# Attention work in three visits per group, with the first block's scores put into the last visit of the group ahead

## The chip, the cores and the metric

The kernel runs on one core of one Trainium2 chip. The metric is the device time of one execution in microseconds, as the median of several runs. The core has five engines that run their own instruction streams in order and meet at semaphores: TensorE (PE; its weight loads are shown apart as PEld), VectorE (DVE), ScalarE (ACT), GpSimd (POOL) and SyncE (SP), which issues the DMAs here.

## The reference

Three stages follow each other over 3072 tokens: a recurrence with decay (8 heads of 48 channels), a feed-forward stage with a quadratic knee, and a gated feed-forward stage.

```python
# stage 1, r k v w: (4, 8, 768, 48)
for t in range(S):
    cur = einsum('bhd,bhe->bhde', u * kt, vt)
    y[:, :, t] = einsum('bhd,bhde->bhe', rt, state + cur)
    state = wt[..., None] * state + einsum('bhd,bhe->bhde', kt, vt)
x = y.transpose(0, 2, 1, 3).reshape(3072, 384)
# stage 2, w_in (384, 2048), w_out (2048, 384)
h = x @ w_in
g = where(h >= 1, h, where(h <= -1, 0, (h + 1) ** 2 / 4))
x = g @ w_out
# stage 3, gate and val (384, 1536), w_out (1536, 384)
g = x @ w_gate
out = (g * sigmoid(g) * (x @ w_val)) @ w_out
```

## The kernel before, in words

Tokens are worked in `NG` = 8 groups of `T` = 384, each group in `NW` = 3 blocks ("windows") of 128 tokens. The recurrence is turned into matrix products per block. For each block there are, on TensorE:

- `AT`, the scores (line 1497): products of k and r, both scaled by running products of w, into two banks. It is one fill of 32 matmuls for a group from the third on, or 28 and more in others.
- `Y`, the output (lines 1523 and 1528): r against the decayed state (32 matmuls, left out for the first block of a sequence), then the masked scores against v (64 matmuls).
- `ST`, the state update (line 1515): k, turned to token order, against v (32 matmuls, 8 in the last block of a sequence).

Every second group begins a sequence, so its first block has no state. For groups 2 to 7 (`moved(g)`, with `MOVED` = 2), k and the output x are turned by VectorE in 32 x 32 blocks and a DMA through DRAM (`turn_k`, `turn_x`, `move_k`, `move_x`), not by TensorE.

The first feed-forward stage is `phase1`: 8 groups of `J1` = 16 slots. In slot j TensorE does `tile_in` for hidden tile j+2 (nine 128x128 by 384 matmuls, line 1438), then the attention work of the next group that is placed in that slot (a "visit"), then `tile_out` for hidden tile j (nine matmuls, line 1466). Each product of fp32 values is three matmuls of a high and a low part. `win_slots(g)` says which attention fills stand in which slot, and TensorE (`do_fill`), ScalarE and VectorE (`drain`) go through them in the same order.

ScalarE computes the knee's first part of tile j+2 (lines 977, 979) and the high part of tile j+1 (970). VectorE makes in slot j the low part of tile j+1 (`lo`, line 1273) and finishes the knee of tile j+2 (`knee`, line 1280). `tile_out(j)` waits for `lo(j)`, and `tile_in(j)` for `knee(j-2)`. After these two VectorE does the slot's other work, placed by tables: the low part of x (`X_SPLIT_SLOTS`, 1268), the turning of k (`K_BLOCK_SLOTS`, `K_BLOCK_AHEAD`, 1251), the scaling of k and r (`SCALE_SLOTS`, `SCALE_AHEAD`, 1153 and 1156), the sums for the term with u (`DIAG_SLOTS`, 1161), the drains of a visit (Y at 1234, x turned at 1260, state at 1223, decay at 1182, masked scores at 1204), and the scans of w for the group after next (`SCAN_SLOTS`, 1131, 1134, 1141). ScalarE checks w in `CHECK_SLOTS`.

GpSimd makes r*k*u for each block (`diag_products`, lines 848 and 851) and, when VectorE has summed it, its product with v (`diag_values`, 858), which the drain of Y adds. SyncE issues loads and moves in one written order (`attention_of`, `half`), and waits at each for what must come before.

A bank written by `ST` has free columns in which the next block's `AT` may stand, so that `AT` needn't wait for the state drain of the same visit; the drain of `ST` then waits for that `AT` fill. Until now this held for the second and third block of a group only.

Phase 2 (8 groups of 12 slots) holds only feed-forward matmuls.

Of the kernel before, what the change touches and what calls it, by code (L numbers as in the profile page):

```python
# [36 lines left out]
NW = 3  # L37
# [25 lines left out]


MOVED = 2
VISITS_MOVED = [[("AT", 0, 0), ("AT", 0, 1)],
                [("Y", 0, 0), ("ST", 0, 0), ("AT", 1, 0), ("AT", 1, 1)],
                [("Y", 1, 0), ("ST", 1, 0), ("AT", 2, 0), ("AT", 2, 1)],
                [("Y", 2, 0), ("ST", 2, 0)]]
FILLS_MOVED = [f for visit in VISITS_MOVED for f in visit]  # L70
NF, NF_MOVED = len(FILLS), len(FILLS_MOVED)
K_BLOCK_SLOTS = {0: 1, 4: 2}
K_BLOCK_AHEAD = {12: 0}
X_SPLIT_SLOTS = {7: 0, 10: 1, 12: 2}
BLK = 32
NB = P // BLK
MOVE = 16 * NB
# [12 lines left out]
OPS_DIAG = 2  # L90


SCALE_SLOTS = {0: 2}
SCALE_AHEAD = {12: 0, 15: 1}
DIAG_SLOTS = {2: 0, 4: 1, 5: 2}
def visits_at(slots, visits, order):
    return {j: tuple(order.index(f) for f in visit) for j, visit in zip(slots, visits)}


WIN_SLOTS = visits_at((1, 3, 6, 8), VISITS_MOVED, FILLS_MOVED)  # L100
WIN_FIRST = visits_at((4, 6, 7, 9, 10, 12, 13), VISITS, FILLS)
XT_FIRST = 13

CHECK_SLOTS = {4: 0, 7: 1, 10: 2}
CHECK_AHEAD_FIRST = {9: 0, 10: 1, 12: 2}
SUM_SLOT = 14
SCAN_SLOTS = {5: 0, 9: 1, 11: 2}


CHECK_FIRST = {0: 1, 3: 2}  # L110
# [12 lines left out]
def first(g):  # L123
    return isinstance(g, int) and g == 0


def win_slots(g):
    return WIN_FIRST if first(g) else WIN_SLOTS


def check_slots(g):
# [19 lines left out]
def fill_no(g, kind, w, n=0):  # L151
    return fills(g).index((kind, w, n))


def build_program(nc, w_d, kr_d, tok_d, u_d, cst_d, w1i_d, w1o_d, w2g_d, w2v_d,
                  w2o_d, rs_d, ks_d, vs_d, ws_d, us_d, out_d, x2_d, ys_d, kb_d, xb_d):
    ctx = ExitStack()
    with ctx:
# [471 lines left out]
        def _(e):  # L630
# [96 lines left out]
            def attention_of(g, loads):  # L727

                def then_load(load, w):
                    if loads:  # L730
                        load(g + 1, w)

                then_load(load_w, 0)
                move_k(g, 1)
                then_load(load_w, 1)
                then_load(load_kr, 0)
                then_load(load_tok, 0)
                move_x(g, 0)
                move_k(g, 2)
                then_load(load_w, 2)  # L740
                move_x(g, 1)
                move_x(g, 2)
                for w in (1, 2):
                    then_load(load_kr, w)
                    then_load(load_tok, w)

            def half(g, after_next):

                if after_next and g == 0:
                    for w in range(NW):  # L750
                        load_kr(2, w)
                        load_tok(2, w)
                elif after_next:
                    attention_of(g + 1, True)
                if after_next:
                    move_k(g + 2, 0)
                wait(M["ea", 1], g * 2 + 4)
                wait(M["ed", 1], g + 2)

                e.dma_start(half_of(x2_d, g), stage[:, :, :]).then_inc(M["st", 1], 16)  # L760
# [56 lines left out]
        @block.gpsimd  # L817
        def _(e):

            e.memset(last[:, :], W_TOT_LEAST).then_inc(zero_p, 1)  # L820
            e.wait_ge(zero_p, 1)
            e.memset(last[:, WIN::SEG], 1.0).then_inc(zero_p, 1)
            e.memset(seed[:, :], 0.0).then_inc(zero_p, 1)
            e.memset(st[:, :, :], 0.0).then_inc(zero_p, 1)
            for i in range(2):
                for n in range(2):
                    e.memset(att[i][n][:, :, :], 0.0).then_inc(zero_p, 1)
            e.memset(sbar[1][:, :, :], 0.0).then_inc(zero_p, 1)
            e.memset(sbar[0][:, :, :], 0.0).then_inc(st_dec, OPS_DECAY)

            def split_lo(c, src, raws, lo, whi_s, wlo_s):
                n = len(raws)
                e.wait_ge(whi_s, c + 1)
                e.wait_ge(raws[c % n], 16 * (c // n + 1))
                e.tensor_tensor(lo[0], src, lo[1].bitcast(F32), ALU.subtract).then_inc(wlo_s, 1)

            def w1_lo(c):
                if c == DVE_CHUNK:
                    return
                t = w1i if c % 2 == 0 else w1o  # L840
                split_lo(c, chunk_raw(c), raw, (t[1][:, c // 2, :], t[0][:, c // 2, :]), whi, wlo)

            def diag_products(g, w):

                n = (g * NW + w) * OPS_DIAG
                rk = r_tok(w)
                e.wait_ge(ld["tok", w], (g + 1) * 16)
                e.tensor_tensor(rk, rk, k_tok(w), ALU.mult).then_inc(diag_p, 1)
                e.wait_ge(diag_p, n + 1)
                e.wait_ge(ld["u"], 16)  # L850
                e.tensor_tensor(rk, rk, uu[:, :], ALU.mult).then_inc(diag_p, 1)

            def diag_values(g, w):

                e.wait_ge(ld["tok", w], (g + 1) * 16)
                e.wait_ge(diag_d, g * NW + w + 1)
                d_b = dg[:, w, :].rearrange("p (h o) -> p h o", o=1).to_broadcast([P, H, D])
                e.tensor_tensor(r_tok(w).rearrange("p (h d) -> p h d", d=D),  # L858
                                v_tok(w).rearrange("p (h d) -> p h d", d=D), d_b, ALU.mult).then_inc(diag_v, 1)

            def decay_second():

                w = 2
                e.wait_ge(scan, OPS_SCAN * w + 1)
                e.wait_ge(st_out, 2 * w)
                e.wait_ge(diag_p, NW * OPS_DIAG)
                for i in range(2):
                    r0, c0 = 64 * i, D * i
                    rows = slice(r0, r0 + D)
                    e.wait_ge(st_dec, OPS_DECAY * w + i * (OPS_DECAY // 2))  # L870
                    wt = suf[rows, w, 0::SEG].rearrange("q (p o) -> q p o", o=1).to_broadcast([D, NPAIR, D])
                    e.tensor_tensor(sbar[twin(0, w)][rows, :, c0:c0 + D], st[rows, :, :], wt, ALU.mult).then_inc(st_dec, OPS_DECAY // 2)
                e.wait_ge(st_dec, OPS_DECAY * (w + 1))

            diag_products(0, 0)
            diag_products(0, 1)
            diag_values(0, 0)
            diag_products(0, 2)
            decay_second()
            diag_values(0, 1)  # L880
            diag_values(0, 2)
            for c in range(2 * J1):
                w1_lo(c)
                if c in PRODUCTS_AT:
                    diag_products(1, PRODUCTS_AT[c])
                if c in VALUES_AT:
                    diag_values(1, VALUES_AT[c])
            for g in range(2, NG):
                for w in range(NW):
                    diag_products(g, w)  # L890
                    diag_values(g, w)
            for c, (j, s) in enumerate(order2):
                lo = w2o[1][:, j, :] if s == 2 else w2gv(1, j, s)
                hi = w2o[0][:, j, :] if s == 2 else w2gv(0, j, s)
                split_lo(c, ring2[:, c % RING2, :], raw2, (lo, hi), whi2, wlo2)
# [226 lines left out]
        def _(e):  # L1122
# [61 lines left out]
            def drain(g, f, parity):  # L1184
# [21 lines left out]
                elif kind == "ST":  # L1206
# [5 lines left out]
                    if moved(g):  # L1212
                        for b in range((n_pair + 1) // 2):
                            if w < NW - 1:
                                e.wait_ge(fill, fills_before(g) + fill_no(g, "AT", w + 1, b) + 1)
                            pairs = slice(2 * b, min(2 * b + 2, n_pair))
                            n_half = pairs.stop - pairs.start
                            for i in range(2):
# [126 lines left out]
            def slot(g, j, parity, next_half, after_next):  # L1345
# [30 lines left out]
                if next_half and not (first(g) and j == XT_FIRST):  # L1376
                    for f in win_slots(g).get(j, ()):
                        drain(g + 1, f, 1 - parity)
                if j == J1 - 1 and first(g):
                    copy_out(1, g)  # L1380
                if after_next:
                    if j in scan_slots(g):
                        scan_window(g + 2, scan_slots(g)[j])
                    if j in SCALE_AHEAD:
                        scale_window(g + 2, SCALE_AHEAD[j])
                    if j in K_BLOCK_AHEAD:
                        turn_k(g + 2, K_BLOCK_AHEAD[j])
                if after_next and j == SUM_SLOT:
                    sum_w(g + 2)
                if j == J1 - 1 and not first(g):  # L1390
# [31 lines left out]
        def _(e):  # L1422
# [114 lines left out]
            def bank_free(g, f):  # L1537

                if moved(g):
                    kind, w, n = fills(g)[f]  # L1540
                    if kind != "Y":
                        e.wait_ge(st_out, states_done(g * NW + w - (1 if kind == "AT" and w > 0 else 0)))
                    if kind == "ST":
                        e.wait_ge(at_out, (g * NW + w + 1) * 2)
                        return
# [50 lines left out]
            def slot(g, j, parity, next_half, after_next):  # L1596
# [10 lines left out]
                if next_half:  # L1607
                    for f in win_slots(g).get(j, ()):
                        do_fill(g + 1, f, 1 - parity)
                tile_out(1, g, j, w1o)  # L1610

            phase1(e, slot)
# [82 lines left out]
```

## Time and profile before

| | us |
|---|---|
| median of 3 runs | 955.07 |
| lowest, highest | 953.28, 956.41 |
| the profiled execution | 953.63 |
| its span, first to last instruction | 951.8 |
| PE busy in it | 933.3 (98%) |
| DVE busy | 548.2 (58%) |
| ACT busy | 392.2 (41%) |
| POOL busy | 173.4 (18%) |

The profiled execution has 1.8 us around its span. Phase 1 with the attention work takes the first half of it (to about 450 us), phase 2 the rest.

How to read the views: "busy" adds up the time in which an engine had an instruction running; "idle before" is the time just before it, with what ended it (the releaser). "issue" is time in which the engine waited for nothing that the profile shows. In the chain of waits each piece is a run of instructions of one line on the path that ended last.

### The profile page before, as it was taken

The page shows a single profiled execution, that of the slowest core. Times are in us where ns is not written, and L with a number is a line of the kernel's source. Part 1 is how long each engine was busy: PE and PEld are TensorE (multiplying, and loading weights), DVE is VectorE, ACT ScalarE, POOL GpSimd, SP SyncE. Part 2 cuts the span into 40 slices and gives each one's busy share as a digit, 9 for nine tenths or more (in the row PEclk, how much of TensorE's full clock was granted, in tenths as well). Part 3 has the DMA queues.
Part 4 walks back from the last instruction along what each step waited for, and adds up shares of the span by engine and source line. Part 5 has one row for each costly group of instructions (what it writes and reads, how often), then busy time and mean ns, then how long its engine had stood idle before and what let it go on. Part 6 is the DMA issues. An engine that isn't in the chain of part 4 may idle for free.

```text
span 951.8 us, 20721 instructions
## 1 busy us (share of the span) xinstructions
PE 933.3 (98%) x8344; PEld 917.5 (96%) x8344; DVE 548.2 (58%) x975; ACT 392.2 (41%) x827; POOL 173.4 (18%) x155
## 2 busy tenths in 40 slices
PE   6899999999999999999999999999999999999998
PEld 5889999999999999999999999999999999999997
DVE  8998877877777778774444433334343343434333
ACT  5675545455554545535664222222222222222222
POOL 6993220402204022021444100000000000000000
PEclk9999999999999999999999999999999999999999
DMA  9824443344433444212324010010101001010000
GB/s 311 247 83 179 139 135 127 113 148 131 142 123 118 142 134 132 110 58 92 108 84 131 3 51 1 1 51 1 51 0 50 0 0 50 0 50 0 25 1 27
DMA packets 49715, 79.58 MB, mean 84 GB/s; under 512 B 14784, under 2 KB 35648, under 8 KB 49632
## 3 DMA queue, kind: packets, MB, share of 16 engines
q1 hardware_dynamic: 49632, 78.42, 25.2%
q8 instruction: 58, 0.95, 0.4%
q14 instruction: 25, 0.20, 0.1%
HBM read 60.71 MB, written 17.69 MB: 82 GB/s over the span
## 4 chain that ended last, share of the span: by engine, by line
PE 93%; DVE 4%; issue 1%; ACT 0%; DMA 0%; DVEq 0%
PE bank L1438 51%; PE bank L1466 36%; PE bank L1497 2%; PE bank L1528 2%; PE bank L1523 1%; DVE suf L1131 1%; PE bank L1515 1%; DVE k_r_by_channel L1156 0%; DVE k_r_by_channel L1153 0%; DVE att L1198 0%; DVE gate L1280 0%; DVE glo L1273 0%; DMA w_by_channel<-in_w_channel 0%; DVE diag L1161 0%; DVE w_by_channel L1141 0%
## 5 line engine op out<-in xcount | busy, mean ns | idle before, releaser
L970 ACT ACTIVATE ghi<-gate 128x384 fp32r<-128x384 f32 x224 | 117.3, 524 | 207.4 <-DVE gate L1292 95.4
L1273 DVE TENSOR_TENSOR glo<-gate,ghi 128x384 fp32r<-128x384 f32 x224 | 136.6, 610 | 83.6 <-ACT ghi L970 81.8
L1290 DVE TENSOR_TENSOR gate<-bank,gate 128x384 f32<-128x384 f32 x96 | 53.5, 558 | 215.0 <-ACT gate L1091 215.0
L1438 PE MATMUL bank<-xhi,w2gv_ahi 128*128 128x384 f32 x480 | 161.3, 336 | 0.0
L1438 PE MATMUL bank<-xlo,w2gv_ahi 128*128 128x384 f32 x480 | 161.3, 336 | 0.0
L1438 PE MATMUL bank<-xhi,w2gv_alo 128*128 128x384 f32 x480 | 161.3, 336 | 0.0
L1091 ACT ACTIVATE gate<-bank 128x384 f32<-128x384 f32 x96 | 47.2, 492 | 227.7 <-PE bank L1438 227.7
L1466 PE MATMUL bank<-ghi,w1ohi 128*128 128x384 f32 x384 | 132.7, 346 | 0.9 <-DVE glo L1273 0.9
L1438 PE MATMUL bank<-xhi,w1ihi 128*128 128x384 f32 x384 | 129.5, 337 | 1.4 <-issue 0.9
L1438 PE MATMUL bank<-xhi,w1ilo 128*128 128x384 f32 x384 | 129.4, 337 | 0.0
L1466 PE MATMUL bank<-glo,w1ohi 128*128 128x384 f32 x384 | 129.4, 337 | 0.0
L1438 PE MATMUL bank<-xlo,w1ihi 128*128 128x384 f32 x384 | 129.2, 337 | 0.0
L1466 PE MATMUL bank<-ghi,w1olo 128*128 128x384 f32 x384 | 129.2, 337 | 0.0
L1280 DVE SCALAR_TENSOR_TENSOR gate<-bank,gate 128x384 f32<-128x384 f32 x128 | 71.0, 555 | 73.4 <-ACT gate L979 72.7
L1466 PE MATMUL bank<-ghi,w2ohi 128*128 128x384 f32 x288 | 96.8, 336 | 0.0
L1466 PE MATMUL bank<-ghi,w2olo 128*128 128x384 f32 x288 | 96.8, 336 | 0.0
L1466 PE MATMUL bank<-glo,w2ohi 128*128 128x384 f32 x288 | 96.8, 336 | 0.0
L977 ACT ACTIVATE gate<-bank 128x384 f32<-128x384 f32 x128 | 62.6, 489 | 82.7 <-PE bank L1438 82.7
L1438 PEld LDWEIGHTS bank<-xhi,w2gv_ahi 128*128 128x128 f32 x480 | 90.2, 188 | 0.0
L1438 PEld LDWEIGHTS bank<-xlo,w2gv_ahi 128*128 128x128 f32 x480 | 90.2, 188 | 0.0
L1438 PEld LDWEIGHTS bank<-xhi,w2gv_alo 128*128 128x128 f32 x480 | 90.2, 188 | 0.0
L858 POOL TENSOR_TENSOR r_k_v_by_token<-r_k_v_by_token,diag 128x384 f32<-128x384 f32 x24 | 27.7, 1155 | 270.9 <-DVE diag L1161 270.8
(105 smaller groups left out, 1550.3 us busy)
## 6 DMA issues: line engine op xcount, KB each, us to landing
r_k_v_by_token<-in_rkv_token SPq DMA_DIRECT2D x21, 672.0 KB, 6.1
k_r_by_channel<-in_kr_channel SPq DMA_DIRECT2D x18, 512.0 KB, 4.9
w_by_channel<-in_w_channel SPq DMA_DIRECT2D x24, 226.2 KB, 3.2
k_blocks_out<-k_blocks SPq DMA_DIRECT2D x18, 256.0 KB, 2.1
k_moved<-k_blocks_out SPq DMA_DIRECT2D x72, 64.0 KB, 2.0
x_t<-ring SPq DMA_DIRECT2D x8, 576.0 KB, 3.2
x_raw<-x_t SPq DMA_DIRECT2D x8, 576.0 KB, 4.0
ring<-in_w_out SPq DMA_DIRECT2D x21, 192.0 KB, 2.8
```

The costliest lines, as they stand in the source:

```text
L858: e.tensor_tensor(r_tok(w).rearrange("p (h d) -> p h d", d=D), v_tok(w).rearrange("p (h d) -> p h d", d=D), d_b, ALU.mult).then_inc(diag_v, 1)
L970: e.activation(ghi[j % 2][:, :], gate[j % 2][:, :], ACT.Copy).then_inc(M["hi", ph], 1)
L977: e.activation(q, hid[j % 2][:, 0:T], ACT.Relu, bias=0.5, scale=0.5).then_inc(M["q", 1], 1)
L1091: e.activation(gate[j % 2][:, :], hid[j % 2][:, 0:T], ACT.Sigmoid).then_inc(M["q", 2], 1)
L1131: e.tensor_tensor_scan(suf[:, w, ::-1], w_at[:, w, :0:-1], last[:, ::-1], 0.0, ALU.mult, ALU.max).then_inc(scan, 1)
L1273: e.tensor_tensor(glo[j % 2][:, :], gate[j % 2][:, :], ghi[j % 2][:, :].bitcast(F32), ALU.subtract)\
L1280: e.scalar_tensor_tensor(q, hid[j % 2][:, 0:T], 1.0, q, ALU.max, ALU.min).then_inc(M["g", 1], 1)
L1290: e.tensor_tensor(q, hid[j % 2][:, 0:T], q, ALU.mult).then_inc(M["t", 2], 1)
L1438: m = e.matmul(out, w_of(a, k), x_of(b_, k), start=start and i == 0, stop=stop and i == total - 1)
L1466: m = e.matmul(acc[k][:, 0:T], wo[a][:, j, k * P:(k + 1) * P], gs[b_][:, :], start=(j == 0 and i == 0), stop=(j == J[ph] - 1 and i == 2))
L1497: m = e.matmul(o[a:a_end, p * WIN + t:(p + 1) * WIN], kr[r, w, 0, p, t:t_end], kr[r, w, 1, p, t:], start=True, stop=True)
L1528: m = e.matmul(out[t, h * D:(h + 1) * D], att[twin(g, w)][h % 2][:, h // 2, t], v_of_scores(g, w, h), start=(row_start and h == 0), stop=( ...
```

## The change

The visits to attention of groups 2 to 7 are placed anew. Before, they stood at slots 1, 3, 6 and 8 of the group ahead: the first scores alone; Y, ST of block 0 with scores 1; Y, ST of block 1 with scores 2; Y, ST of block 2. Now they stand at slots 2, 5 and 8, and the scores of the first block of groups 3 to 7 follow Y and ST of the last block of the group before them, in its visit at slot 8. Group 2 has no such visit ahead, so its first scores stand alone, at slot 0 instead of slot 1.

Around it:
- the drain of `ST` of a group's third block waits for the next group's first `AT`, and that `AT` no longer for the third block's state drain (`joined`);
- the scaling, the turning and the move of the first block's k come earlier: slot 6 and 7 instead of 12, and on SyncE between the moves of x of blocks 1 and 2 instead of at the end;
- the third block's scaling is at slot 1 (was 0), the sums at 1, 3, 6 (were 2, 4, 5), the splits of x at 6, 9, 12 (were 7, 10, 12), the checks at 3, 7, 10 (were 4, 7, 10), the scans at 4, 10, 13 (were 5, 9, 11);
- GpSimd makes all three blocks' products of a group before the first of its values.

```diff
-VISITS_MOVED = [[("AT", 0, 0), ("AT", 0, 1)],
-                [("Y", 0, 0), ("ST", 0, 0), ("AT", 1, 0), ("AT", 1, 1)],
+FIRST_SCORES = [("AT", 0, 0), ("AT", 0, 1)]
+VISITS_MOVED = [[("Y", 0, 0), ("ST", 0, 0), ("AT", 1, 0), ("AT", 1, 1)],
                 [("Y", 1, 0), ("ST", 1, 0), ("AT", 2, 0), ("AT", 2, 1)],
                 [("Y", 2, 0), ("ST", 2, 0)]]
-FILLS_MOVED = [f for visit in VISITS_MOVED for f in visit]
+FILLS_MOVED = FIRST_SCORES + [f for visit in VISITS_MOVED for f in visit]
-K_BLOCK_AHEAD = {12: 0}
-X_SPLIT_SLOTS = {7: 0, 10: 1, 12: 2}
+K_BLOCK_AHEAD = {7: 0}
+K_BLOCK_AHEAD_FIRST = {12: 0}
+X_SPLIT_SLOTS = {6: 0, 9: 1, 12: 2}
-SCALE_SLOTS = {0: 2}
-SCALE_AHEAD = {12: 0, 15: 1}
-DIAG_SLOTS = {2: 0, 4: 1, 5: 2}
+SCALE_SLOTS = {1: 2}
+SCALE_AHEAD = {6: 0, 15: 1}
+SCALE_AHEAD_FIRST = {12: 0, 15: 1}
+DIAG_SLOTS = {1: 0, 3: 1, 6: 2}
-WIN_SLOTS = visits_at((1, 3, 6, 8), VISITS_MOVED, FILLS_MOVED)
+WIN_SLOTS = visits_at((2, 5, 8), VISITS_MOVED, FILLS_MOVED)
+WIN_SECOND = {0: (0, 1), **WIN_SLOTS}
+SCORES_AHEAD = 8
-CHECK_SLOTS = {4: 0, 7: 1, 10: 2}
+CHECK_SLOTS = {3: 0, 7: 1, 10: 2}
-SCAN_SLOTS = {5: 0, 9: 1, 11: 2}
+SCAN_SLOTS = {4: 0, 10: 1, 13: 2}
...
+def scores_ahead(g, j):
+    return g + 1 >= MOVED and g + 2 < NG and j == SCORES_AHEAD
...
@@ SyncE, attention_of(g, loads)
                 move_x(g, 1)
+                if loads:
+                    move_k(g + 1, 0)
                 move_x(g, 2)
...
@@ GpSimd
             for g in range(2, NG):
                 for w in range(NW):
                     diag_products(g, w)
+                for w in range(NW):
                     diag_values(g, w)
...
@@ VectorE, drain of ST
                             if w < NW - 1:
                                 e.wait_ge(fill, fills_before(g) + fill_no(g, "AT", w + 1, b) + 1)
+                            elif g + 1 < NG:
+                                e.wait_ge(fill, fills_before(g + 1) + fill_no(g + 1, "AT", 0, b) + 1)
...
@@ VectorE, slot
+                if scores_ahead(g, j):
+                    for n in range(2):
+                        drain(g + 2, fill_no(g + 2, "AT", 0, n), parity)
...
@@ TensorE, bank_free
-                        e.wait_ge(st_out, states_done(g * NW + w - (1 if kind == "AT" and w > 0 else 0)))
+                        joined = kind == "AT" and g * NW + w > MOVED * NW
+                        e.wait_ge(st_out, states_done(g * NW + w - (1 if joined else 0)))
...
@@ TensorE, slot
+                if scores_ahead(g, j):
+                    for n in range(2):
+                        do_fill(g + 2, fill_no(g + 2, "AT", 0, n), parity)
```

## Rows read from the trace of the kernel before

**Rows 1.** The profile's page: span, busy time of each engine, and 40 slices.
```profile
span 951.8 us, 20721 instructions
PE 933.3 (98%) x8344; PEld 917.5 (96%) x8344; DVE 548.2 (58%) x975; ACT 392.2 (41%) x827; POOL 173.4 (18%) x155
...
PE   6899999999999999999999999999999999999998
```

**Rows 2.** Chain of waits, main groups 5 and 6: start us, us, what.
```profile
357.17 0.80 PE bank L1523 x32
...
359.11 0.84 PE bank L1497 x22
359.95 1.77 PE bank L1466 x9
...
368.34 1.76 PE bank L1466 x9
...
396.62 0.81 PE bank L1497 x24
397.43 1.78 PE bank L1466 x9
```

**Rows 3.** Chain of waits, from main group 2's last visit to group 3's first.
```profile
188.35 1.56 PE bank L1438 x9
189.91 0.80 PE bank L1523 x32
...
193.38 1.59 PE bank L1438 x9
...
218.81 1.59 PE bank L1438 x9
...
223.01 1.56 PE bank L1438 x9
```

**Rows 4.** Chain of waits, main group 1's visit at slot 6.
```profile
122.52 0.70 PE bank L1497 x15
123.22 0.51 issue
123.73 0.55 PE bank L1497 x10
```

**Rows 5.** DMA queues in the window from 119 to 126 us: packets, MB, share of engines.
```profile
q8 instruction: 2, 0.03, 1.9%
```

**Rows 6.** TensorE in order of time, main group 4: visits at 3 and 8 begin.
```profile
286.02 0.87 PE L1523 MATMUL bank<-state_decayed,k_r_by_channel 112*32 112x96 f32 x32
...
307.62 0.87 PE L1523 MATMUL bank<-state_decayed,k_r_by_channel 112*32 112x96 f32 x32
```

**Rows 7.** VectorE in order of time, main group 4, slots 3 to 7.
```profile
287.68 0.55 DVE L1234 TENSOR_TENSOR x_by_token<-bank,r_k_v_by_token 128x384 f32<-128x384 f32 x1
...
292.32 0.54 DVE L1273 TENSOR_TENSOR glo<-gate,ghi 128x384 fp32r<-128x384 f32 x1
...
293.82 0.70 DVE L1251 STREAM_TRANSPOSE k_blocks<-k_r_by_channel 128x512 f32<-128x512 f32 x1
...
295.12 1.22 DVE L1273 TENSOR_TENSOR glo<-gate,ghi 128x384 fp32r<-128x384 f32 x1 [0.17 <-ACT ghi L970]
...
298.34 0.55 DVE L1161 TENSOR_REDUCE diag<-r_k_v_by_token 128x8 f32<-128x384 f32 x1 [1.32 <-POOL r_k_v_by_token L851]
298.81 1.22 DVE L1131 TENSOR_TENSOR_SCAN suf<-w_by_channel,last_of_segment 112x516 f32<-112x516 f32 x1
...
301.67 0.53 DVE L1273 TENSOR_TENSOR glo<-gate,ghi 128x384 fp32r<-128x384 f32 x1
...
306.97 0.54 DVE L1273 TENSOR_TENSOR glo<-gate,ghi 128x384 fp32r<-128x384 f32 x1
```

**Rows 8.** GpSimd in order of time, main group 3: the value of block 0.
```profile
226.85 1.24 POOL L858 TENSOR_TENSOR r_k_v_by_token<-r_k_v_by_token,diag 128x384 f32<-128x384 f32 x1 [40.56 <-DVE diag L1161]
```

**Rows 9.** SyncE's DMA issues in order of time, main group 2: block 2's k.
```profile
182.61 3.02 SPq L684 DMA_DIRECT2D k_moved<-k_blocks_out  x4
```

More of the change, by code:

```diff
@@ L127, in win_slots @@
 def win_slots(g):
-    return WIN_FIRST if first(g) else WIN_SLOTS
+    return WIN_FIRST if first(g) else WIN_SECOND if g + 1 == MOVED else WIN_SLOTS
+def scores_ahead(g, j):
+    return g + 1 >= MOVED and g + 2 < NG and j == SCORES_AHEAD
 def check_slots(g):
@@ L754, in half @@
                     attention_of(g + 1, True)
-                if after_next:
-                    move_k(g + 2, 0)
+                if after_next and g == 0:
+                    move_k(2, 0)
                 wait(M["ea", 1], g * 2 + 4)
@@ L1383, in slot @@
                         scan_window(g + 2, scan_slots(g)[j])
[L1384 to L1387, printed above, removed]
+                    scale_ahead = SCALE_AHEAD_FIRST if first(g) else SCALE_AHEAD
+                    if j in scale_ahead:
+                        scale_window(g + 2, scale_ahead[j])
+                    k_ahead = K_BLOCK_AHEAD_FIRST if first(g) else K_BLOCK_AHEAD
+                    if j in k_ahead:
+                        turn_k(g + 2, k_ahead[j])
                 if after_next and j == SUM_SLOT:
```

## The prediction, made before the changed kernel was timed

> **What bounds the kernel now.** I read the page first, then the chain of waits through phase 1, then single visits in order of time. TensorE is busy for 933.3 of 951.8 us, and its row of slices is full from the third slice on [rows 1]. What is missing, 18.5 us, lies almost all in the first 45 us, which the change doesn't touch. So no other engine is the bound. A change to the placing of attention work can gain only in three ways: less lost time where TensorE goes from one kind of tile to another, fewer stalls inside a visit, or a shorter pitch of the large matmuls. In the chain of waits a tile of nine large matmuls takes 1.56 us, and a visit is the same few pieces each time, 0.80 for r against the state and 0.84 for scores among them [rows 2, 3]. Two things in the chain depart from this pattern: stretches in which a tile takes 1.59 us instead of 1.56 [rows 3], and one visit with 0.51 us of "issue" in the middle of its scores [rows 4].
>
> **One visit less.** The first scores cost, alone, their piece of 0.81 us plus a longer first tile after them, 1.78 against 1.56: 0.81 + 0.22 = 1.03 us [rows 2, 3]. The visits with Y pay that longer first tile in any case: 1.76 without scores at the end, 1.77 with them [rows 2]. Joined scores so add 0.84 + 0.01 = 0.85 us. Each join saves 1.03 - 0.85 = **0.18 us**, and there are five (groups 3 to 7): 0.9 us. Group 2's first scores only go from slot 1 to slot 0: nothing gained. The matmuls themselves are all still there. (The Trainium skill, page "TensorEngine Tiling (Array Packing)", section "Key Properties", says that changing the tiling mode drains TensorE. The trace agrees in sign: a join takes away one such change, and 0.18 us is what that is worth here.)
>
> **The pitch.** After main group 2's last visit all 17 tiles up to group 3's first visit take 1.59 us; before the visit, and after the next one, 1.56 [rows 3]. The same happens after group 4's last visit, and for five tiles after the visits at slot 3 in groups 1 and 2: some 44 tiles at 0.03 us, 1.3 us in all. Nothing waits in these tiles. It looks like a phase in which TensorE comes out of a visit and which it keeps until the next. The two long stretches both follow a last visit that ends with ST, two of the six such visits; of the eighteen visits that end in scores two were followed by a slow stretch, a short one. After the change five of the six last visits end in scores. If they come out like those, the two long stretches go: 2 x 17 x 0.03 = **1.0 us**. At 2 in 18 over five stretches of 20 tiles some 0.3 us of that comes back. I take 0.7 us. Bounds: all five slow costs 5 x 20 x 0.03 = 3.0 us against the 1.0 of now, a loss of 2.0; all short stretches fast as well gains 1.3.
>
> **The stall.** Group 1's scores at slot 6 took 0.70 + 0.51 + 0.55 = 1.76 us for 0.84, with no semaphore between their matmuls [rows 4], while instruction blocks and k's small packets were under way [rows 5]. I read it as TensorE waiting for its instructions. The same visit exists after the change, now at slot 5, so I leave it where it is: 0. It can go (a gain of 0.92) or come at other visits (below).
>
> **VectorE.** It loses no work and gets none: its operations change place. The question is where `lo` or `knee` now comes late. After visit 5 is the narrowest place. Take the start of visit 2 as zero and use main group 4's times around its visit at slot 3, which began at 286.02. The drains run from 287.68 to 292.32, that is from +1.7 to +6.3 [rows 6, 7]. In slot 4 the knee of tile 6 is bound by TensorE: `tile_in(6)` ends at 2.8 + 4 x 1.56 + 0.2 = +9.2, and with ScalarE's checks (now in slot 3) the knee is done by about +11.0. The turning of k (0.70) and a scan (298.81 to 301.67, 2.86) follow: +14.6 [rows 7]. With `lo`, `knee` +15.5. The drains of visit 5, 4.64 long: +20.1, then `lo(7)` +20.6. TensorE wants it after two visits of 2.8, ten tiles and twice 0.2: +21.6. So there is 1.0 us to spare. In the kernel before, the like place is after the visit at slot 6: `lo(8)` ended at 307.5, when `tile_in(10)` was just over, and only the visit at slot 8, which began at 307.62, covered it [rows 6, 7]. There VectorE had also waited 1.32 us for GpSimd's product of block 2 [rows 7]; as the products now come before all values, that wait goes. I cost VectorE at 0, covered by 1.0 us after visit 5; from both sides, it can't gain (no wait of TensorE on VectorE is there to remove after 50 us), and each us beyond the cover costs 6 us, one for each group.
>
> After visit 2 `lo(4)` is done by +6.8 and wanted at 2.8 + 0.2 + 4 x 1.56 = +9.2. After visit 8 the drains may first start at +1.6 past its start, `lo(10)` follows at +6.8 and is wanted at +9.2; the scan in slot 10 comes behind it. Both have 2.4 us of cover. At slot 13 the scan stands without k's scaling and turning, which were at 12, so it is no worse than slot 11's now. The scores ahead need k scaled at slot 6: the scaling ends near +23, the scores start near +26.6.
>
> **GpSimd and the sums.** The sum of block 0 moves to slot 1 behind a scaling, ending near zero; GpSimd's value takes 1.24 [rows 8], and the drain of Y wants it at +1.6. That is 0.3 us of cover, with visit 2's 2.4 us behind it. The products of block 2, now queued ahead of the first value, wait for its load, which is issued after x's third move and has some 20 us. (The Trainium skill, page "SBUF — State Buffer", section "SBUF: two separate sides", says that a VectorE operation with two SBUF inputs and a GpSimd operation lock each other out. The trace agrees: a `lo` beside GpSimd took 1.22 us for 0.54 [rows 7]. By that rule every overlap would be worth up to 0.7 us on VectorE, within the cover.)
>
> **SyncE's queue.** The move of block 0's k of the next group now stands ahead of x's third move. It waits for k turned at slot 7 (near +25) and the moved block takes some 4 us from store to the last load; x's third block is turned near +28. Nothing waits behind it yet. In slot distance x's moves have 3 slots and more as before. The third k move follows x's first: in group 2 its loads were issued at 182.61, and the visit at slot 8 that wants them began at 189.91 [rows 3, 9]. From the first visit with Y to that at slot 8 there were five slots and are now six, so its 7.3 us grow by one slot's 3.1. The turning at slot 7, which needs the k buffer free, has about one slot less, some 4 us after the move has landed. Cost 0, covered by that.
>
> **The sum.** 953.63 (951.8 of span and 1.8 around it) - 0.9 - 0.7 = 952.0 for an execution like the profiled one. The median of the three runs lies 1.44 above that execution, so the same change puts the median at 955.07 - 1.6 = **953.4 us**, 0.17% less.
>
> **Rivals.**
> - *Instructions come late at visit 8.* With the scores it has up to 160 matmuls and as many weight loads in 2.8 us, where before it had 128 or fewer pairs. Visits of that size are the ones where the stall [rows 4] happened, once in nine. (The Trainium skill, page "Runtime: NRT & Kernel Launch", section "Instruction fetch mechanics", says that instructions come in blocks of 256; a visit of 320 may cross two blocks. The two instruction packets in that window agree [rows 5].) If all five visits stall for 0.92 us: +4.6 - 1.6 = +3.0, that is 958.1, **slower**. It decides against the change from the second stall on (0.92 x 2 > 1.6). For it: the next group's k now moves at that time, too. Against: eight of nine such visits had none.
> - *VectorE comes late after visit 5.* If the cover of 1.0 is short by 0.3 to 0.8, 6 x = 1.8 to 4.8 us: 955.2 to 958.2.
> - *The pitch goes the wrong way.* All five stretches slow: 955.07 - 0.9 + 2.0 = 956.2.
> - *More goes than I count.* The stall of group 1 (0.92) and all slow stretches (1.3) go with the 0.9: 955.07 - 3.1 = 952.0, **faster** by over 0.3%.
> - *Nothing changes:* joined scores cost what lone ones did, since the free time is that of the bank switch, and the pitch stays: 955.1.
>
> **How the numbers follow.** 0.3% of 955.07 is 2.9 us, about what a measurement of this kernel can tell from none: below 952.2 is faster, above 957.9 slower. The forecast (a gain of 0.9 to 2.4 us) has 0.52, instructions late 0.09, VectorE late 0.10, pitch worse 0.09, more gained 0.12, nothing 0.08. The three runs differ by 3.1 us, which spreads each case by some 1 us: faster takes half of its rival's case and a fifth of the forecast, 0.19; slower takes most of the first and half of the second rival, 0.12; 0.69 for within. The range reaches down to the fourth rival with that spread and up to the first two: 951.2 to 957.2.
>
> **What would show it.** Right: in groups 3 to 7 no scores alone; the piece of scores after ST at slot 8 at 0.81 to 0.85 us with a next tile of 1.76 to 1.79; tiles of 1.56 from visit 8 to visit 2; no wait of TensorE on VectorE after 50 us. Wrong: "issue" within a visit, a wait of line 1466 on `glo` (1273) in slot 7 or of 1438 on the gate (1280), 1.59 us over the long stretches, or a lone 1.3 us of POOL's wait now on VectorE's sums at slot 2.

## The result, and the profile after

| | before | after |
|---|---|---|
| median of 20 runs | 955.08 us | 957.71 us |
| lowest, highest | 952.66, 957.62 | 954.65, 961.05 |
| ratio after to before (95% interval) | | 1.0026 (1.0017 to 1.0035) |
| the profiled execution, its span | 953.63, 951.8 us | 958.64, 956.9 us |

The changed kernel is slower by 2.6 us, where 1.7 us less was forecast. The time lies 0.5 us above the range, whose end was 957.2.

The page has nearly the same busy times as before [rows 1]:

```profile
span 956.9 us, 20723 instructions
PE 935.7 (98%) x8344; PEld 921.0 (96%) x8344; DVE 556.7 (58%) x975; ACT 393.3 (41%) x827; POOL 171.5 (18%) x155
```

The view that settles it is that of the waits of TensorE alone, from 95 to 460 us. Columns: us in total, times, longest. Of the kernel before, the one line was the stall of [rows 4]:

```profile
PE bank L1497 <- issue: 0.5, 1, 0.5
```

After:

```profile
PE bank L1515 <- issue: 3.0, 3, 1.1
```

The matmuls wait for no other engine there; TensorE stops three times in the middle of scores, for "issue". The chain of waits shows them at slot 5 of main group 2, slot 2 of group 4 and slot 8 of group 5:

```profile
180.44 0.81 PE bank L1515 x22
181.25 1.02 issue
182.27 0.27 PE bank L1515 x2
...
286.34 0.83 PE bank L1515 x23
287.17 1.07 issue
288.24 0.33 PE bank L1515 x3
...
370.98 0.82 PE bank L1515 x21
371.80 0.94 issue
372.75 0.34 PE bank L1515 x5
```

Undisturbed, a visit with state, scores, ST and the next scores takes 3.32 us from the start of the last matmul of `tile_in` to that of the second of `tile_out`. These three took 4.58, 4.71 and 4.59: 3.9 us lost, against 0.9 in the one of before (4.24). That is 3.0 us more. The joins stand where they should. Here is the one of main group 4, slot 8, with what follows it:

```profile
311.93 0.20 PE bank L1533 x7
312.13 0.83 PE bank L1515 x24
312.96 1.80 PE bank L1484 x9
314.76 1.59 PE bank L1456 x9
...
343.38 1.59 PE bank L1456 x9
...
348.91 1.56 PE bank L1456 x9
```

The scores add their 0.83 us and no second change of tiles, but all 19 tiles from there to the next visit go at 1.59 us, as 17 did behind group 2 before [rows 3]. In this execution some 66 tiles did so (19 each after groups 4 and 5, 23 after group 6, 5 in group 3), 2.0 us in all, against 1.3 before. From the visit after them on (348.91) a tile takes 1.56 us again.

The two spans differ by 5.1 us: 3.0 of stalls, -0.9 of joins, +0.7 of pitch, and 2.4 us that the first 50 us took longer (the first visit of group 1's attention came at 50.66 instead of 48.22), where both kernels have the same work. That last part differs from execution to execution: the first large tile began at 28.88 in the profile of before and at 30.45 in this one; over the profiles below it lay between 28.9 and 30.0 us, in no order that I can see (but for the one with 140 increments). Without it there remain 2.8 us, and the medians differ by 2.6.

### The profile page after: what moved, and what is told of

Same layout as the page of the kernel before. It is cut to its first block, busy times and chain, and to the rows that moved or that the text cites. A ratio compares the mean times of both kernels' runs of the same rounds, so it can differ in the third digit from the quotient of the medians.

```text
span 956.9 us, 20723 instructions
## 1 busy us (share of the span) xinstructions
PE 935.7 (98%) x8344; PEld 921.0 (96%) x8344; DVE 556.7 (58%) x975; ACT 393.3 (41%) x827; POOL 171.5 (18%) x155
## 4 chain that ended last, share of the span: by engine, by line
PE 93%; DVE 3%; issue 1%; DMA 1%; ACT 1%; SPq 0%; DVEq 0%; ACTq 0%
PE bank L1456 51%; PE bank L1484 36%; PE bank L1515 2%; PE bank L1546 2%; PE bank L1541 2%; PE bank L1533 1%; DMA w_by_channel<-in_w_channel 1%; DVE suf L1142 1%; DVE gate L1293 0%; DVE glo L1286 0%; PE bank L1501 0%; ACT state_decayed L940 0%; DVE k_r_by_channel L1167 0%; DVE w_by_channel L1152 0%; DVE k_r_by_channel L1164 0%
## 5 line engine op out<-in xcount | busy, mean ns | idle before, releaser
L1286 DVE TENSOR_TENSOR glo<-gate,ghi 128x384 fp32r<-128x384 f32 x224 | 141.2, 630 | 82.1 <-ACT ghi L981 80.6
L1484 PEld LDWEIGHTS bank<-ghi,w1ohi 128*128 128x128 f32 x384 | 72.1, 188 | 3.9 <-issue 2.2
```

What stands on the lines that cost most here:

```text
L1286: e.tensor_tensor(glo[j % 2][:, :], gate[j % 2][:, :], ghi[j % 2][:, :].bitcast(F32), ALU.subtract)\
L1484: m = e.matmul(acc[k][:, 0:T], wo[a][:, j, k * P:(k + 1) * P], gs[b_][:, :], start=(j == 0 and i == 0), stop=(j == J[ph] - 1 and i == 2))
```

## Theory and rivals

**Theory: instruction blocks.** All three stalls, and the one of before, have the same place in TensorE's instruction stream. Counting its instructions in the trace (weight loads, matmuls and the few semaphore instructions), they come behind numbers 4544, 7104, 9408 and, before, 3008. All four leave 192 when divided by 256. Over phase 1 of the profile of after the instruction queue moves one packet of 16 KB for each 256 of TensorE's instructions. (The Trainium skill, page "Runtime: NRT & Kernel Launch", section "Instruction fetch mechanics", gives 16 KiB blocks of 256 instructions; the trace agrees. It also says that crossing a boundary is mostly hidden, as instructions are issued more slowly than fetched. In these visits that isn't so: 327 instructions pass in 2.8 us, and the stalls above are measured.) A visit with Y, ST and scores has 327 instructions, so that two ends of blocks can lie in it. The positions of the first end in the four stalled visits were 45 (before), 64, 62 and 58 instructions from the visit's start; the next end comes 256 later, and there the stall is. In two visits of before, groups 2 and 4, the first end stood at 28 and 26, and nothing stalled. My reading: the block after next is asked for when one ends; if that is at the start of a visit, it was asked for while the large matmuls still ran, and if it is deeper in, the 256 instructions of the next block are used up in 2 us, before the new one is there. The instruction packets bear this out: in the three stalled visits they began 0.5, 0.7 and 0.4 us after that end (0.5 in the one of before), in the two unstalled ones 0.9 and 1.2 us ahead of it. From the first end to the end of the stall it took 3.2 to 3.3 us in the three visits of after and 2.8 in that of before. Two views of the DMA queues (packets, MB, share of engines) show it: the stalled visit of after at 178 us has its first end at 179.05, and the packet comes in the 2 us behind it (window from 179.05 to 181.05):

```profile
q8 instruction: 1, 0.02, 4.6%
```

The unstalled visit of before at 181 us has its first end at 180.85, and the packet comes in the 2 us ahead (window from 178.85 to 180.85; the 2 us behind have none):

```profile
q8 instruction: 1, 0.02, 3.0%
```

The visit that stalls is thus a matter of the program's layout, which added or moved instructions change. The joins move it, and three more visits have 327 instructions (twelve instead of nine).

**Rivals.** The new places in the slots cost the time, by waits or pitch. Or: the stalls belong to DMA traffic at that moment. Or: the pitch of 1.59 us is worse since the visits end otherwise.

The theory allows a test that leaves every piece of work in place: put some instructions ahead of TensorE's first fill, where it waits for its first data anyway, and shift all the ends of blocks. Increments of a semaphore that nothing waits for serve as such.

## Experiment 1: the changed kernel, shifted by 62

```diff
+            for _ in range(62):
+                e.sem_inc(HELD["pe"], 1)
             for f in range(NF):
                 do_fill(0, f, 0)
```

> The changed kernel with 62 semaphore increments put ahead of TensorE's first fill; nothing else. Theory (instruction blocks): TensorE's instructions come in blocks of 256, and TensorE stops inside a visit when one block ends 35 to 70 instructions into it and the next ends 256 later, still in the visit. The 62 instructions move every boundary, and no visit is left with two of them in that position: the three stalls of 1.21 to 1.34 us at 181, 287 and 371 us go (3.8 us less), no 'issue' within a visit after 95 us, and the median falls from 957.7 to about 954, 1.1 us below the kernel before. Rival (the placing): the new slots cost it, through waits or the pitch; then the stalls stay in the same visits or the time stays within 1 us of 957.7.

Measured: median 953.25 us (12 runs) against 955.12 of the kernel before on the same chip, ratio 0.9984 (0.9976 to 0.9993). The three stalls are gone, and the changed kernel is now faster than the one before. Group 3's last visit, with its joined scores, in the chain of waits:

```profile
247.38 0.80 PE bank L1541 x32
248.18 0.68 PE bank L1546 x64
248.86 0.45 PE bank L1533 x31
249.31 0.84 PE bank L1515 x22
250.16 1.77 PE bank L1484 x9
```

The new places of the work thus cost next to nothing; the rival of the placing falls. One trace of VectorE's lateness is left: in main group 3, slot 7, TensorE waited for `lo(7)`, and its large matmuls there came 0.26 us late, in this one of the six profiles of the changed kernel:

```profile
PEld bank L1484 <- DVE glo L1286: 0.4, 1, 0.4
```

Behind the 62 increments the first matmul came at 10.7 us, where the changed kernel has it at 7.7, so they outlast TensorE's wait for its first data by 3.0. The first large tile still began at 29.39 us, between the 28.88 and 30.45 of the two kernels without increments, so what was lost at the start was made up by then.

The waits of the weight loads showed a small rest, at two visits with a block's end 77 and 79 instructions in, whose next end lies just behind the visit; the tiles there came 0.25 and 0.37 us late:

```profile
PEld bank L1484 <- issue: 0.9, 2, 0.5
```

## Experiments 2 and 3: the kernel before, shifted by 20 and by 140

Same edit in the kernel before, with `range(20)` and `range(140)`.

> The kernel before with 20 semaphore increments ahead of TensorE's first fill. Theory (instruction blocks): its one stall, 0.78 us at 123 us, goes, since the boundary moves from 45 to 25 instructions into that visit and no other visit comes into the position: no 'issue' within a visit, median 0.8 us below the kernel before, 954.3. Rival: a stall belongs to the DMA traffic of that moment; it stays where it is.

Measured: 953.99 us, ratio 0.9993 (0.9984 to 1.0002), 1.1 us lower by the medians. There was no stall in any visit. The interval reaches 1, so the time alone would not show it; the trace does.

> The kernel before with 140 semaphore increments ahead of TensorE's first fill. Theory (instruction blocks): boundaries now fall some 64, 58 and 41 instructions into the visits of main group 2 at slot 3, group 5 at slot 6 and group 6 at slot 6, with the next 256 later: three stalls of about 1.3, 1.2 and 0.7 us there, none at 123 us, and the median rises by 2 to 2.5 us over the kernel before, to 957.3, although every placing is that of before. Rival (the placing of the change is what costs): no change beyond 0.5 us.

Measured: 968.19 us, ratio 1.0148 (1.013 to 1.0165): 13 us more, not 2.5. The increments cost far more than I thought. TensorE's first matmul came behind them:

```profile
PE bank L1486 <- issue: 22.6, 1, 22.6
```

That is 0.16 us for each, and it goes on past the 7 us in which TensorE waits for its first data. The first large tile came at 40.9 us instead of 28.9, and 12 of the 13 us are this. The rest of the trace is as expected: stalls at 182, 371 and 430 us, in the three visits named, and none at 123:

```profile
PE bank L1497 <- issue: 1.5, 3, 0.7
```

As a measure of the stalls' price this run says nothing, which is why it was made again with a smaller shift.

## Experiment 4: the kernel before with three stalls

The kernel before with `range(55)`.

> The kernel before with 55 semaphore increments ahead of TensorE's first fill: few enough that they lie within TensorE's wait for its first data (62 of them did not move the first large tile, 140 did by 10 us). Theory (instruction blocks): boundaries 67, 50 and 48 instructions into the visits at slot 6 of main groups 3 and 4 and at slot 3 of group 6, each with the next one 256 later: three stalls of about 1.2, 0.9 and 0.9 us in those visits, none at 123 us; the median rises by 2 us, to 957.2, the level of the changed kernel. Rival (placing): no change.

Measured: 956.08 us against 954.24 of before on that chip, ratio 1.0022 (1.0012 to 1.0033), 1.8 us more. With every piece of work where it was, the kernel before is now within reach of the changed one (1.0026). The stalls stand in the three visits named, for example that of group 4, slot 6:

```profile
300.16 0.70 PE bank L1497 x17
300.86 1.47 issue
302.33 0.44 PE bank L1497 x8
```

The visits took 0.8, 1.8 and 1.4 us longer than one without a stall, 4.0 us in all in that execution and 3.1 more than the one stall of before; the median rose by 1.8. The size of a stall varies, between 0.8 and 1.8 us over this study, though its place doesn't. Against the same kernel with 17 increments (953.04 us, on the same chip, below), which has no stall, it is 3.0 us more.

## Experiments 5 and 6: the pair without stalls

The changed kernel with `range(54)` and the kernel before with `range(17)`.

> The changed kernel with 54 increments instead of 62. With 62, three visits had a block end 77 to 79 instructions in, and the next 6 to 8 instructions behind the visit, and there the tile behind two of them came 0.2 to 0.4 us late. Theory (instruction blocks): with 54 the nearest positions are 27, and 85 to 89, outside the range that stalls; these waits of line 1484 go too, and the median is 0.5 us below that of the one with 62, some 952.8 against 955.1 of before. Rival: they had another cause and stay, same median as with 62.

> The kernel before with 17 increments: boundaries 28 and 86 to 88 instructions into its visits, none in the range that stalls. Theory: no stall in any visit after 95 us; it stands against the changed kernel with 54 increments as the pair without stalls, and what is left between them is the five joins, 0.9 us, give or take the pitch of the stretches: 954.0 against 953.0.

Measured on one chip, 12 runs each: the kernel before 954.24, before shifted by 17 **953.04**, ratio 0.9988 (0.9979 to 0.9997), changed and shifted by 54 **952.28**, ratio 0.9978 (0.9967 to 0.9989). No visit of either stalled, and the two small waits of line 1484 were gone. Between the two lie 0.76 us, where the joins were costed at 0.9. The changed kernel with 62 and the kernel before with 20, on another chip, lay 0.74 us apart the same way. The intervals of the ratios overlap in both pairs, so the traces must carry it. In group 5's visit at slot 8 of the changed kernel:

```profile
366.37 0.48 PE bank L1533 x31
366.85 0.81 PE bank L1515 x24
367.67 1.77 PE bank L1484 x9
```

0.81 us for the scores and the same 1.77 behind them that a visit without them has [rows 2]. The version of 952.28 us has the lowest median of this study, below both kernels.

## Experiment 7: the changed kernel without the join

```diff
-    return WIN_FIRST if first(g) else WIN_SECOND if g + 1 == MOVED else WIN_SLOTS
+    return WIN_FIRST if first(g) else WIN_SECOND if g + 1 >= MOVED else WIN_SLOTS
...
-    return g + 1 >= MOVED and g + 2 < NG and j == SCORES_AHEAD
+    return False
...
-                        joined = kind == "AT" and g * NW + w > MOVED * NW
+                        joined = kind == "AT" and w > 0
```

and without the wait of the state's drain for the next group's scores, with the 62 increments.

> The changed kernel with the first block's scores alone at slot 0 of every group instead of joined at slot 8 of the group ahead (visits at 0, 2, 5 and 8), everything else in the new slots, and the 62 increments. Theory: boundaries put no visit at risk (no stall), and five lone visits of scores cost 1.03 us where the joined ones cost 0.85: the median is 0.9 us above that of a62, about the kernel before with 20 increments. Rival (the join is worth nothing): same as a62. Rival (the new slots cost something by themselves): above the kernel before.

Measured: 953.59 us, ratio 0.9984 (0.9973 to 0.9995), 0.34 above the changed kernel shifted by 62, on the same chip. The direction is the expected one, the size isn't resolved (the two intervals are 0.2% wide). The trace has each lone visit at the price it had before:

```profile
276.15 0.81 PE bank L1513 x24
276.97 1.78 PE bank L1482 x9
```

1.03 us by the same sum as for [rows 2]. So by the traces five joins are worth 0.9 us on TensorE's path. In its profile the joined kernel gave back 0.6 of this in the small waits of experiment 1 and 0.26 in the wait for VectorE. This one has two visits with a block's end at the same 77 and 79, and no such waits; why is open.

## Experiment 8: how deep a block's end must lie

The changed kernel with `range(30)`.

> The changed kernel with 30 increments: a graded test of where a block may end. Boundaries fall 51, 34, 32 and 28 instructions into the visits at slot 5 of main groups 1 and 2, slot 2 of group 4 and slot 8 of group 5, each with the next 256 later. Theory: a stall needs the first boundary so deep in the visit that its block is asked for late: about 0.9 us at 51, 0.0 to 0.4 at 34 and 32, none at 28; median about 1 us above the changed kernel with 62 increments, some 954. Rival (any visit with two boundaries stalls in full): four stalls of over 0.9, median 957.

Measured: 953.28 us (10 runs), ratio 0.9987 (0.9977 to 0.9998), 1.0 us above the one with 54 increments on the same chip. The visit with the first end at 51 stalled, in the chain of waits:

```profile
120.86 0.70 PE bank L1515 x18
121.56 1.20 issue
122.76 0.44 PE bank L1515 x6
```

The visits at 34, 32 and 28 did not stall at all. So it isn't enough that a visit holds two ends. All visits of 327 instructions in the twelve profiles of this study, by where the first end of a block lies in them (counted in the traces; us from the last matmul of `tile_in` to the second of `tile_out`):

| first end, instructions into the visit | visits | us each |
|---|---|---|
| 0 to 34 | 25 | 3.31 to 3.36 |
| 42 to 67 | 14 | 4.08 to 5.12 |
| 77 to 79 | 4 | 3.31 to 3.32 (in one kernel 0.2 to 0.4 us lost in the tile behind) |
| 81 to 255 | 83 | 3.31 to 3.47 |

There is no exception on either side. The instruction packets divide the visits in the same way. In the 25 visits of the first row the packet began 0.3 to 2.1 us ahead of the block's end; in the 14 stalled ones it began 0.3 to 1.3 us behind it, and work came back 2.3 to 2.9 us after the packet had begun. Most of the spread in size comes from that beginning: the three longest losses, 1.5 to 1.8 us, had it 0.7 to 1.3 us behind, the three shortest, 0.8 us, 0.3 to 0.4.

## Experiments 9 and 10: the same programs once more

The changed kernel, and the one shifted by 54, without any edit.

> The changed kernel once more, unchanged. Theory (instruction blocks, a matter of the program's layout): the same three visits stall again, those at slot 5 of main group 2, slot 2 of group 4 and slot 8 of group 5, by 1.2 to 1.4 us each in all. The slow pitch of 1.59 us: if it, too, belonged to the layout, it would stand after the same visits (slot 8 of main groups 4, 5 and 6, slot 5 of group 3); if it is chance, after others.

> The changed kernel with 54 increments once more. Theory: no stall in any visit again. The pitch of 1.59 us stood after two visits, short stretches (297 and 355 us); by chance it would stand elsewhere now, by layout at the same ones.

Measured: 959.13 us and 951.68 us, one run each, beside 952.84 of before. The stalls came at the same three visits of the changed kernel (178, 284 and 370 us) and at none of the shifted one. The slow pitch did not: it stood after slot 8 of group 2 and slot 2 of group 5 in the one, and after slot 8 of group 6 in the other, at none of the places of the first time. So the stalls belong to the program, the places of the pitch to the execution.

The second profile of the changed kernel shows one thing more. Behind the stall at 287 us, the tiles are long:

```profile
287.10 1.34 issue
288.44 0.33 PE bank L1515 x3
288.76 2.70 PE bank L1484 x9
291.47 2.19 PE bank L1456 x9
293.66 1.56 PE bank L1484 x9
```

The view by windows has the clock (columns: stretch, its length and the busy times, then the granted clock):

```profile
287.00:289.00 2.00, 0.66 (x8) 0.49 (x5) 0.37 (x2) 0.00 (x0) 0.00 (x0) 1.00 0.66 189
289.00:293.00 4.00, 4.00 (x16) 4.00 (x15) 3.39 (x9) 0.53 (x1) 0.00 (x0) 0.57 0.89 304
293.00:296.00 3.00, 3.00 (x19) 3.00 (x18) 1.02 (x2) 2.24 (x6) 0.06 (x1) 1.00 0.12 34
```

After 1.34 us without work TensorE was granted 0.57 of its clock from 289 to 293 us, that is mostly the lower level, 1.2 GHz, with 0.32 us from matmul to matmul instead of 0.17. The two tiles cost 2.70 - 1.76 + 2.19 - 1.56 = 1.6 us on top of the stall. That may be why the changed kernel's slowest runs reach 961 us. Two of its three slowest, 961.05 and 960.16 us, list a mean granted clock of 0.998 where most have 0.999 or 1.0, but the third, 960.61, has 0.999. The lower clock inside the span is seen in one profile only, so how often it happens stays open.

## Why the prediction was wrong, point by point

**What bounds the kernel** held: TensorE's matmuls wait for no other engine between 95 and 460 us in either kernel.

**One visit less** held: 0.83 to 0.85 us for joined scores, 1.03 alone, 0.9 us for five.

**The stall** is the step that failed. I wrote "The same visit exists after the change, now at slot 5, so I leave it where it is: 0." I took it for a thing of that visit. It belongs to the position of the visit in the instruction stream, and the change moves every position behind it. That visit came through unharmed (its first end went from 45 to 81), and three others stalled, for 3.9 us instead of 0.9. The term that I put at 0 measured +3.0 us.

**The first rival** had the mechanism, and its price each, and named the point from which it decides. But I gave it five visits at slot 8, all or none, and 0.09. The better question was at which number in its stream each visit begins. A range of 26 to 42 positions of 256 stalls (42 to 67 for certain, 35 to 76 at most), so of twelve visits of 327 instructions one or two were to be expected, and three were hit; only one of them was a visit at slot 8 with the new scores. The positions could have been counted from the trace of before: with 45 stalling and 28 and 26 not, the rule was nearly there. I had divided one stall by nine visits and called that a chance.

**The pitch** I costed at 0.7 us gained; in the profile it was 0.7 lost. It isn't tied to places in the program: over the twelve profiles of this study a slow stretch followed 22 of 216 visits that end in scores and 10 of 42 that end in ST, and it came back at none of its places in the two programs that were profiled twice. If these rates hold, the change makes it a little rarer in the mean, an estimate of some 0.3 us, and one profile says nothing on that. The places of before were drawn by chance, and I counted them as a property of the kernel. What starts a slow stretch is open.

**VectorE** held in the changed kernel. `lo(7)` of group 4 ended at 305.73 and `tile_out(7)` began at 307.17, 1.4 us later, where I had worked out 1.0:

```profile
305.19 0.54 DVE L1286 TENSOR_TENSOR glo<-gate,ghi 128x384 fp32r<-128x384 f32 x1
```

The place was rightly named as the narrowest: the one wait for VectorE in all six profiles of the changed kernel stood there, 0.26 us (experiment 1).

**GpSimd, SyncE** held: VectorE waited 0.3 us once for GpSimd's value in the drain of Y, where I had 0.3 us of cover, and 0.5 us once for the move of x.

**The sum**: with -0.9 for the joins, +3.0 for the stalls, and the pitch left at zero in the mean, 955.1 + 2.1 = 957.2 against 957.7 measured; the interval of the ratio is 1.6 to 3.3 us. The instructions' part alone turned the sign.

Not tried: what makes an instruction packet begin later in one stalled visit than in another (0.3 to 1.3 us behind the block's end), DMA traffic of that moment for one. That the block after next is asked for when one ends is my reading of these times; no run shows it by itself.

## What to carry to other kernels

On an engine that is always busy, look up where its stalls of kind "issue" stand in its own instruction stream, counted from the start: if their numbers leave the same rest when divided by the block's size, they belong to the layout, and a few instructions without effect, put where the engine waits anyway, move them away. Compare two kernels only after this is done on both, since a change that moves instructions can bring a gain or loss by chance that has nothing to do with its merit: here the kernel before alone had medians of 953.0, 954.2 and 956.1 us on one chip with 17, 0 and 55 increments, and a change worth -0.8 us measured +2.6. And don't count a slow stretch or a stall of one profile into a sum before knowing whether it comes back.

## What the runs showed of the hardware that I had not expected

- Bursts of small matmuls can outrun TensorE's supply of instructions: 256 passed in 2.0 us, and from the end of one block to the return of work it took 2.7 to 3.7 us in the fourteen stalls, 2.3 to 2.9 of them from the start of the instruction packet.
- A semaphore increment on TensorE's stream costs 0.15 to 0.16 us when many stand in a row (the first matmul came at 22.6 us behind 140, at 10.7 behind 62 and at 9.5 behind 54).
- Large matmuls of 384 columns run in one of two lasting rhythms, 0.173 us apart, or 0.179 and 0.174 in turn (1.56 and 1.59 us for nine), entered on leaving a visit, at other places in each execution.
- A stall of 1.34 us was followed once by some 3.5 us mostly at the lower clock (granted 0.57 over 4 us); none of the other thirteen stalls was.
